# One run of the V products instead of two halves in a fused attention and mixer kernel

## The chip, the cores and the metric

The kernel runs on one core of a Trainium2 chip. The metric is the device time of one execution in microseconds (us), the median over several executions. Short names for the engines: PE is TensorE (PEld its weight loads), DVE is VectorE, ACT is ScalarE, POOL is GpSimd, SP is SyncE. The memories are SBUF and, for what PE writes, the eight banks of PSUM.

## The reference

Attention over 32 heads (batch 4, 8 heads, 576 tokens, head size 64) with a threshold below each row's largest score, then a token mixer and a channel mixer, then a gated convolution layer. The change touches attention alone:

```python
scores = scale * np.matmul(q, k.transpose(0, 1, 3, 2))
thresh = np.max(scores, axis=-1, keepdims=True) - tau
scores = np.where(scores >= thresh, scores, -1000000000.0)
scores = scores - np.max(scores, axis=-1, keepdims=True)
attn = np.exp(scores)
attn = attn / (np.sum(attn, axis=-1, keepdims=True) + 1e-09)
return np.matmul(attn, v).astype(np.float32)
...
x = _moe_ref(x=x, **moe_kwargs)
return _moe2_ref(x=x, **moe2_kwargs)
```

## The kernel before

Every engine has a program of its own, written out by hand, and semaphores tie them together; no planner moves anything. In the first 390 us or so attention and the token mixer are computed, in the rest the channel mixer and the last layer.

Attention goes through 16 pairs of heads. The program calls `body` for k = 0 to 17: body k works on the scores and probabilities of pair k, on the V products of pair k-1 (`at.pv`, k = 1 to 16), and on the token mixer of pair k-2 (`at.mix`, k = 2 to 17). A body has five steps s = 0 to 4, one for each tile of 128 queries; the fifth tile holds the last 64 queries of both heads.

What PE does in step s, in this order: `scores` of the tile two ahead (L979, L981), `turn_probs` of tile s (L998, L1006: the masked probabilities are transposed in pieces into two PSUM banks, `score` 3 and `turn_y`; the second head's pieces wait for that head's mask), `times_v` (L1035, in steps 0 and 1 only), `turn_tails` (L1017), `times_v_tail` (L1045, step 1), token mixer work (steps 2 to 4: L1080, L1089, L1102; L1052 and L1062 turn attention's output), and `score_tails` of the tile three ahead (L967, L970).

`score_tails` writes into the PSUM banks from which DVE reads the scores, so it waits for `max_done`: DVE must have copied the tile before it. DVE does in step s `copy_out` of the tile two ahead (L817: one operation for each head, from PSUM to `negs`, with the row's minimum) and then `mask` of the tile one ahead (L834: one for each head, `negs` and `exps` to `prob`). ACT copies the turned probabilities to SBUF (L596) and takes exponentials (L584). POOL splits arrays into two parts for precise products: `h1h`, `h1l` (L447, L495), `xh`, `xl` (L447, L474), adds `uy` (L502), and splits a piece of a weight, `w1h`, `w1l` (L454, L485); it starts that sequence in step 4, when ACT has written `h1f` (L632). PE's `mix_out` (L1102) in step 4 waits for `h1l`.

`times_v` multiplies the four key tiles of 128 keys (FULL = 4) by V. For each key tile it issues two products of 288 queries (bank `out_t` and bank `mixed`) for each of two heads. Its waits stand ahead of key tile 0 alone.

Of the kernel before, what the change touches and what calls it, by code (L numbers as in the profile page):

```python
# [25 lines left out]
def build(nc, q, k, v, v_tail, tau, w_tok1, w_tok2, w_ch1, w_ch2, w_in, conv_w, w_out, out):  # L26
# [10 lines left out]
    FULL = S // P  # L37
# [155 lines left out]
    with ctx:  # L193
# [763 lines left out]
        def _(pe):  # L957
# [14 lines left out]
            def scores(unit):  # L972

                g, k, t = unit
                par = k % 2
                if t < FULL:
                    for h in range(2):
                        rows = slice(h * D, (h + 1) * D)
                        mm = nc.tensor.matmul(score[:, 2 * h, :], qT[par][rows, t * P:(t + 1) * P], kT[par][rows, 0:MAIN])  # L979
                else:  # L980
                    mm = nc.tensor.matmul(score[:, 0, :], qd[par][:, :], kT[par][:, 0:MAIN])  # L981
                mm.then_inc(s_done, 1)

            def turn_probs(at, t):
                g, k = at.g, at.k
                i = slot_of(k, t)
                if NT * k + t >= 1:
                    pe.wait_ge(turn_drained, 2 * (NT * g + t))
                if t < FULL:
                    for h in range(2):  # L990
                        pe.wait_ge(mask_done, tiles_to(g, t) + h + 1)
                        pe.nop(nofuse=True)
                        for kt in range(FULL):
                            k_at = h * (S + TAIL) + kt * P
                            to = (h * FULL + kt) * D
                            for r in range(2):
                                rows = slice(r * D, (r + 1) * D)
                                mm = nc.tensor.transpose(turn[r][:, to:to + D], prob[rows, i, k_at:k_at + P],  # L998
                                                         ident[rows, rows])
                else:  # L1000
                    pe.wait_ge(mask_done, TILES * (g + 1))
                    pe.nop(nofuse=True)
                    for kt in range(FULL):
                        for r in range(2):
                            rows = slice(r * D, (r + 1) * D)
                            nc.tensor.transpose(turn[r][:, kt * D:(kt + 1) * D], prob[rows, i, kt * P:(kt + 1) * P],  # L1006
                                                ident[rows, rows])
                    to = slice(FULL * D, NT * D)
                    nc.tensor.transpose(turn[0][0:TAIL, to], prob[0:D, i, MAIN:S], ident[0:D, 0:D])
                    mm = nc.tensor.transpose(turn[1][:, to], prob[D:P, i, S - P:S], ident[D:P, D:P])  # L1010
                mm.then_inc(t_done, 1)

            def turn_tails(at, t):
                g, k = at.g, at.k
                if t == 0 and k >= 2:
                    pe.wait_ge(xt_drained, g - 1)
                nc.tensor.transpose(tails[:, t * P:(t + 1) * P], prob[:, slot_of(k, t), MAIN:MAIN + 2 * TAIL], ident[:, :]) \  # L1017
                    .then_inc(tail_turned, 1)

            def times_v(pair, k, kts):  # L1020

                par = k % 2
                if kts[0] == 0:
                    pe.wait_ge(v_loaded[par], V_LOADS * (pair // 2 + 1))
                    pe.wait_ge(turn_drained, 2 * NT * (pair + 1))
                    if k >= 1:
                        pe.wait_ge(x_done, pair)
                        pe.wait_ge(short_x, pair)
                    if k >= 2:
                        pe.wait_ge(u_drained, 2 * (pair - 1))  # L1030
                for kt in kts:
                    for c, bank in enumerate((out_t, mixed)):
                        for h in range(2):
                            mine = slice(h * D, (h + 1) * D)
                            nc.tensor.matmul(bank[mine, 0:HALF], vm[par][:, kt, mine],  # L1035
                                             probT[par][:, h, kt, c * HALF:(c + 1) * HALF],
                                             start=(kt == 0), stop=False, skip_group_check=True)

            def times_v_tail(pair, k):
                par = k % 2  # L1040
                pe.wait_ge(tails_drained, pair + 1)
                if k < 2:
                    pe.wait_ge(set_once, 5)
                for c, bank in enumerate((out_t, mixed)):
                    mm = nc.tensor.matmul(bank[:, 0:HALF], vd[par][:, :], probTt[par][:, c * HALF:(c + 1) * HALF],  # L1045
                                          start=False, stop=True, skip_group_check=True)
                mm.then_inc(pv_done, 1)

            def turn_out(pair):
                pe.wait_ge(out_drained, 2 * (pair + 1))  # L1050
                for t in range(FULL):
                    mm = nc.tensor.transpose(out_t[:, t * P:(t + 1) * P], oT[:, t * P:(t + 1) * P], ident[:, :])  # L1052
                mm.then_inc(xa_done, 1)

            def turn_out_tail(pair):
                nc.tensor.transpose(mixed[:, DT:DT + P], oT[:, MAIN:MAIN + 2 * TAIL], ident[:, :]).then_inc(xa_tail_done, 1)
# [8 lines left out]
            def mix_hidden(pair, k):  # L1065

                if k == 0:
                    pe.wait_ge(wt_split, 3)
                pe.wait_ge(x_split, pair + 1)
                if k < PAIRS - 1:  # L1070
                    pe.wait_ge(out_drained, 2 * (pair + 2))
                else:
                    pe.wait_ge(u_drained, 2 * pair)
                pe.nop(nofuse=True)
                nc.tensor.transpose(mixed[:, DT:DT + TAIL], x32[0:TAIL, FULL, :], ident[0:TAIL, 0:TAIL])
                n = 0
                for kt in range(NT):
                    w = width[kt]
                    for x, wt in ((xh, wt1h), (xh, wt1l), (xl, wt1h)):
                        mm = nc.tensor.matmul(mixed[:, 0:DT], x[0:w, kt, :], wt[0:w, kt, :],  # L1080
                                              start=(n == 0), stop=(n == 3 * NT - 1))
                        n += 1
                mm.then_inc(tok_done, 1)

            def turn_hidden(pair):
                pe.wait_ge(relu_done, pair + 1)
                pe.wait_ge(xt_tail_drained, pair + 1)
                for m in range(KT):
                    mm = nc.tensor.transpose(mixed[:, m * P:(m + 1) * P], h1T[:, m * P:(m + 1) * P], ident[:, :])  # L1089
                mm.then_inc(hT_done, 1)  # L1090
# [53 lines left out]
            def body(at):  # L1144
                g, k = at.g, at.k
                for s in range(NT):
                    two, three = at.unit(s + 2), at.unit(s + 3)
                    if two:
                        scores(two)
                    if at.units:  # L1150
                        turn_probs(at, s)
                    if at.pv and s < 2:
                        times_v(g - 1, k - 1, (2 * s, 2 * s + 1))
                    if at.units and s < FULL:
                        turn_tails(at, s)
                    if at.pv and s == 1:
                        times_v_tail(g - 1, k - 1)
                    if at.mix and s == 2:
                        mix_hidden(g - 2, k - 2)
                        if k == PAIRS + 1:  # L1160
                            hidden(2)
                    if s == 3:
                        if at.mix:
                            turn_hidden(g - 2)
                        if at.pv:
                            turn_out(g - 1)
                            turn_out_tail(g - 1)
                        if k >= PAIRS:
                            hidden(3 * (k - PAIRS))
                    if at.pv and s == 4:  # L1170
                        turn_x(g - 1, k - 1)
                    if at.mix and s == 4:
                        mix_out(g - 2, k - 2)
                        if k == PAIRS:
                            hidden(1)
                    if three:
                        score_tails(three)
# [29 lines left out]
            with pe.Fori(0, B // 2) as j:  # L1207
                for par in range(2):
# [16 lines left out]
                    for kt in range(KF):  # L1225
                        pe.wait_ge(wo_split, kt + 1)
                        pe.wait_ge(z_lo, KF * b + kt + 1)
                        for t in range(FULL):
                            at = slice(t * P, (t + 1) * P)
# [37 lines left out]
```

## Time and profile before

| | |
|---|---|
| median of 3 executions | 900.53 us (900.35 to 900.69) |
| profiled execution | 903.3 us, of which the span of its instructions is 901.5 us |
| PE busy in the span | 849.2 us, 94% |
| DVE, ACT, POOL busy | 430.0, 411.2, 277.9 us |
| mean granted clock of PE | 0.988 of full speed |

The span is the time from the first to the last instruction. A busy time is the time in which at least one instruction of that engine is in flight; PE's matmuls overlap one another, and their ends are modelled.

### The profile page before, as it was taken

The page shows a single profiled execution, that of the slowest core. Times are in us where ns is not written, and L with a number is a line of the kernel's source. Part 1 is how long each engine was busy: PE and PEld are TensorE (multiplying, and loading weights), DVE is VectorE, ACT ScalarE, POOL GpSimd, SP SyncE. Part 2 cuts the span into 40 slices and gives each one's busy share as a digit, 9 for nine tenths or more (in the row PEclk, how much of TensorE's full clock was granted, in tenths as well). Part 3 has the DMA queues.
Part 4 walks back from the last instruction along what each step waited for, and adds up shares of the span by engine and source line. Part 5 has one row for each costly group of instructions (what it writes and reads, how often), then busy time and mean ns, then how long its engine had stood idle before and what let it go on. Part 6 is the DMA issues. An engine that isn't in the chain of part 4 may idle for free.

```text
span 901.5 us, 15052 instructions
## 1 busy us (share of the span) xinstructions
PE 849.2 (94%) x5536; PEld 667.2 (74%) x5536; DVE 430.0 (48%) x839; ACT 411.2 (46%) x866; POOL 277.9 (31%) x218
## 2 busy tenths in 40 slices
PE   4789989999999999979999999999999999999998
PEld 1456666666666666667888888888899989899996
DVE  4877766777777777452121121121121736438290
ACT  2677767777777777532111121121111746447371
POOL 2323332333333333341201010030066463708170
PEclk9799999999999999989999999999999999999999
DMA  7311111111111111300000000000041001010101
GB/s 210 96 44 43 43 45 43 42 42 42 42 42 42 42 42 15 140 1 1 1 0 1 1 1 1 0 1 1 1 152 36 2 1 47 1 58 0 47 0 58
DMA packets 30890, 32.19 MB, mean 36 GB/s; under 512 B 12352, under 2 KB 19072, under 8 KB 30848
## 3 DMA queue, kind: packets, MB, share of 16 engines
q1 hardware_dynamic: 30848, 31.61, 11.8%
q8 instruction: 28, 0.46, 0.2%
q14 instruction: 14, 0.11, 0.0%
HBM read 26.88 MB, written 4.72 MB: 35 GB/s over the span
## 4 chain that ended last, share of the span: by engine, by line
PE 87%; ACT 4%; issue 3%; DVE 2%; POOL 2%; SPq 0%; DMA 0%; ACTq 0%; POOLq 0%; DVEq 0%
PE score L1122 17%; PE score L1218 11%; PE score L979 6%; PE out_t L1137 4%; PE turn_y L1137 4%; PE mixed L1137 4%; PE tails L1137 4%; PE out_t L1035 4%; PE mixed L1080 4%; PE out_t L1203 4%; PE mixed L1035 3%; PE score L998 3%; PE turn_y L1203 2%; PE mixed L1203 2%; PE tails L1203 2%
## 5 line engine op out<-in xcount | busy, mean ns | idle before, releaser
L817 DVE TENSOR_SCALAR_CACHE_REDUCE negs<-score,neg_scale 128x576 f32<-128x576 f32 x144 | 112.7, 816 | 99.7 <-PE score L979 69.7
L895 DVE SCALAR_TENSOR_TENSOR h<-score,h 128x512 fp32r<-128x512 f32 (+1 forms) x60 | 38.3, 638 | 241.7 <-ACT h L676 241.7
L676 ACT ACTIVATE h<-score 128x512 fp32r<-128x512 f32 (+1 forms) x60 | 33.3, 555 | 255.8 <-PE score L1122 255.8
L834 DVE SCALAR_TENSOR_TENSOR prob<-negs,thresh,exps 128x576 f32<-128x576 f32 x144 | 143.1, 1025 | 0.3 <-ACT thresh L587 0.3
L584 ACT ACTIVATE exps<-negs,neg_max 128x576 f32<-128x576 f32 x144 | 104.9, 776 | 6.8 <-DVE negs L817 6.4
L1122 PE MATMUL score<-uh,w1h 128*128 128x512 f32 (+1 forms) x240 | 89.5, 373 | 3.2 <-DVE ul L865 3.2
L1122 PE MATMUL score<-ul,w1h 128*128 128x512 f32 (+1 forms) x240 | 89.1, 371 | 0.0
L1122 PE MATMUL score<-uh,w1l 128*128 128x512 f32 (+1 forms) x240 | 89.0, 371 | 0.0
L552 POOL TENSOR_TENSOR zl<-z,zh 128x512 fp32r<-128x512 f32 x32 | 54.9, 1715 | 98.1 <-ACT zh_t L750 98.1
L979 PE MATMUL score<-kT,qT 64*128 64x512 f32 x256 | 78.9, 695 | 0.0
L998 PEld LDWEIGHTS score<-ident,prob 64*128 64x128 f32 x512 | 43.2, 144 | 45.5 <-issue 45.4
L596 ACT ACTIVATE probT<-score 128x512 f32<-128x512 f32 x64 | 38.2, 598 | 83.6 <-PE turn_y L998 83.6
L447 POOL TENSOR_SCALAR h1h<-h1f 128x256 fp32r<-128x256 f32 x16 | 7.5, 467 | 216.0 <-ACT h1f L632 216.0
L510 POOL TENSOR_TENSOR ul<-uy,uh 128x256 fp32r<-128x256 f32 (+6 forms) x7 | 16.7, 2403 | 173.9 <-ACT uh L663 173.9
L935 DVE SCALAR_TENSOR_TENSOR conv<-hpad,cw,conv 128x576 f32<-128x576 f32 x32 | 27.3, 854 | 77.4 <-ACT conv L763 77.4
L1218 PE MATMUL score<-yl,wih 128*128 128x288 f32 x256 | 54.9, 296 | 0.0
L1218 PE MATMUL score<-yh,wih 128*128 128x288 f32 x256 | 54.8, 296 | 0.0
L1218 PE MATMUL score<-yh,wil 128*128 128x288 f32 x256 | 54.8, 296 | 0.0
L1122 PEld LDWEIGHTS score<-uh,w1h 128*128 128x128 f32 x240 | 45.8, 191 | 11.1 <-issue 3.4
L998 PE MATMUL score<-ident,prob 64*128 64x64 f32 x512 | 47.3, 229 | 4.5 <-DVE prob L834 3.8
L1122 PEld LDWEIGHTS score<-ul,w1h 128*128 128x128 f32 x240 | 45.9, 191 | 7.7
L1122 PEld LDWEIGHTS score<-uh,w1l 128*128 128x128 f32 x240 | 45.7, 191 | 7.7
(184 smaller groups left out, 2050.3 us busy)
## 6 DMA issues: line engine op xcount, KB each, us to landing
qT<-in_q SPq DMA_DIRECT2D x16, 288.0 KB, 2.9
kT<-in_k SPq DMA_DIRECT2D x16, 288.0 KB, 3.0
vm<-in_v SPq DMA_DIRECT2D x16, 256.0 KB, 2.7
result<-ostage SPq DMA_DIRECT2D x16, 256.0 KB, 2.1
w1f<-in_moe_w_ch SPq DMA_DIRECT2D x4, 768.0 KB, 9.2
w2f<-in_moe_w_ch SPq DMA_DIRECT2D x4, 768.0 KB, 7.8
wif<-in_moe_w_in SPq DMA_DIRECT2D x1, 2048.0 KB, 7.8
wof<-in_moe_w_out SPq DMA_DIRECT2D x8, 256.0 KB, 2.5
```

What stands on the lines that cost most here:

```text
L552: nc.gpsimd.tensor_tensor(zl[:, t, :], z32[:, t % 2, 0:MAIN], zh[:, t, :].bitcast(F32), ALU.subtract)
L584: nc.scalar.activation(exps[i][:, h, :], negs[:, i, h, :], ACT.Exp, bias=neg_max[:, i, h:h + 1], scale=-1.0).then_inc(exp_done, 1)
L817: nc.vector.tensor_scalar(negs[:, i, h, :], raw_of[h], neg_scale[:, 0:1], None, ALU.mult, ALU.min, accum_out=neg_max[:, i, h:h + 1]).then_ ...
L834: nc.vector.scalar_tensor_tensor(out=prob[:, i, h * S:(h + 1) * S], in0=negs[:, i, h, :], scalar=thresh[:, i, h:h + 1], in1=exps[i][:, h, ...
L895: nc.vector.scalar_tensor_tensor(out=h3[:, n % RING, 1, 0:w], in0=hidden_banks[n % 4][:, 0:w], scalar=0.0, in1=h3[:, n % RING, 0, 0:w].bit ...
L979: mm = nc.tensor.matmul(score[:, 2 * h, :], qT[par][rows, t * P:(t + 1) * P], kT[par][rows, 0:MAIN])
L998: mm = nc.tensor.transpose(turn[r][:, to:to + D], prob[rows, i, k_at:k_at + P], ident[rows, rows])
L1035: nc.tensor.matmul(bank[mine, 0:HALF], vm[par][:, kt, mine], probT[par][:, h, kt, c * HALF:(c + 1) * HALF], start=(kt == 0), stop=False, s ...
L1122: mm = nc.tensor.matmul(hidden_banks[n % 4][:, 0:w], wt[:, c, kt, :], x[:, kt, 0:w], start=(kt == 0 and i == 0), stop=(kt == KM - 1 and i ...
L1137: mm = nc.tensor.matmul(sum_banks[mt][:, 0:w], wt[:, c, o:o + P], h3[:, n % RING, part, 0:w], start=(c == 0 and i == 0), stop=(c == KC - 1 ...
L1203: mm = nc.tensor.matmul(bank, z, wt[:, kt, :], start=(kt == 0 and n == 0), stop=(kt == KF - 1 and n == 2))
L1218: mm = nc.tensor.matmul(in_banks[c % 2][:, i, 0:HALF], wt[:, kt, c * P:(c + 1) * P], y[:, kt, i * HALF:(i + 1) * HALF], start=(n == 0), st ...
```

## The change

In the body's steps on PE, `times_v` is called once in step 1 with all four key tiles, where it was called in step 0 with the first two and in step 1 with the last two. The products and their number are the same.

```diff
                     if at.units:
                         turn_probs(at, s)
-                    if at.pv and s < 2:
-                        times_v(g - 1, k - 1, (2 * s, 2 * s + 1))
+                    if at.pv and s == 1:
+                        times_v(g - 1, k - 1, range(FULL))
                     if at.units and s < FULL:
                         turn_tails(at, s)
                     if at.pv and s == 1:
```

The instructions of the other four engines keep their order. On PE, steps 0 and 1 of one body (k = 3) stand so before the change; `kd`, `kT`, `qT`, `qd` are the operands of the scores, `ident` with `prob` a transposition of probabilities, `vm` is V, and a row with a wait names the semaphores. Left-out rows are the other pieces of the transpositions and of the V products.

```order
L979 MATMUL score<-kT_69,qT_67 128x512 x2
L998 MATMUL score<-ident,prob 128x64 [waits turn_drained,mask_done]
...
L1035 MATMUL out_t<-probT_77,vm_75 64x288 [waits short_x,x_done,u_drained,turn_drained,v_loaded0]
...
L1017 MATMUL tails<-ident,prob 128x128 [waits xt_drained]
L967 MATMUL score<-kd_84,qT_67 128x2x64 [waits max_done]
L979 MATMUL score<-kT_69,qT_67 128x512 x2
L998 MATMUL score<-ident,prob 128x64 [waits turn_drained,mask_done]
...
L1035 MATMUL out_t<-probT_77,vm_75 64x288 x2
...
L1017 MATMUL tails<-ident,prob 128x128
L1045 MATMUL out_t<-probTt_74,vd_76 128x288 [waits tails_drained]
```

And so after it, the same steps of the same body, with the same rows left out:

```order
L979 MATMUL score<-kT_69,qT_67 128x512 x2
L998 MATMUL score<-ident,prob 128x64 [waits turn_drained,mask_done]
...
L1017 MATMUL tails<-ident,prob 128x128 [waits xt_drained]
L967 MATMUL score<-kd_84,qT_67 128x2x64 [waits max_done]
L979 MATMUL score<-kT_69,qT_67 128x512 x2
L998 MATMUL score<-ident,prob 128x64 [waits turn_drained,mask_done]
...
L1035 MATMUL out_t<-probT_77,vm_75 64x288 [waits short_x,x_done,u_drained,turn_drained,v_loaded0]
...
L1017 MATMUL tails<-ident,prob 128x128
L1045 MATMUL out_t<-probTt_74,vd_76 128x288 [waits tails_drained]
```

The first eight products have moved from between the transpositions of tile 0 and its `tails` to the place behind the transpositions of tile 1, and the five waits of key tile 0 moved with them. The row with `waits max_done` now follows the transpositions of tile 0 with only `tails` in between.

## Rows read from the trace of the kernel before

**Rows 1.** The page: span and busy times, slices of PE's granted clock in tenths.

```profile
span 901.5 us, 15052 instructions
...
PE 849.2 (94%) x5536; PEld 667.2 (74%) x5536; DVE 430.0 (48%) x839; ACT 411.2 (46%) x866; POOL 277.9 (31%) x218
...
PEclk9799999999999999989999999999999999999999
```

**Rows 2.** Busy time by stretch, sum over the five steps of one pair.

```profile
sum 22.55, PE 21.07 PEld 14.10 DVE 16.44 ACT 16.02 POOL 7.66; mean PE 4.21 PEld 2.82 DVE 3.29 ACT 3.20 POOL 1.53
```

**Rows 3.** Waits of that pair, 222.22 to 244.77 us: total, times, longest.

```profile
DVE negs L817 <- PE score L979: 4.1, 3, 2.5
...
PE out_t L1102 <- POOL h1l L495: 1.3, 1, 1.3
```

**Rows 4.** Timeline, PE, steps 0 and 1 of that pair: start, duration, instruction.

```profile
223.78 0.71 PE L1035 MATMUL out_t<-probT,vm 128*64 128x288 f32 x4
...
225.87 0.33 PE L1017 MATMUL tails<-ident,prob 128*128 128x128 f32 x1
226.03 0.39 PE L967 MATMUL score<-kd,qT 128*128 128x128 f32 x2
226.35 1.13 PE L979 MATMUL score<-kT,qT 64*128 64x512 f32 x4
227.31 0.22 PE L998 MATMUL score<-ident,prob 64*128 64x64 f32 x1
...
227.77 0.24 PE L998 MATMUL score<-ident,prob 64*128 64x64 f32 x1
...
228.16 0.71 PE L1035 MATMUL out_t<-probT,vm 128*64 128x288 f32 x4
...
229.67 0.66 PE L1035 MATMUL mixed<-probT,vm 128*64 128x288 f32 x4
230.25 0.33 PE L1017 MATMUL tails<-ident,prob 128*128 128x128 f32 x1
```

**Rows 5.** Timeline, DVE, the same steps.

```profile
223.40 0.82 DVE L817 TENSOR_SCALAR_CACHE_REDUCE negs<-score,neg_scale 128x576 f32<-128x576 f32 x1 [1.43 <-PE score L979]
...
224.88 0.08 DVE L817 DVE_READ_ACCUMULATOR negs<-score,neg_scale 128x1 f32 x1
224.88 1.26 DVE L834 SCALAR_TENSOR_TENSOR prob<-negs,thresh,exps 128x576 f32<-128x576 f32 x1
...
226.07 1.54 DVE L834 SCALAR_TENSOR_TENSOR prob<-negs,thresh,exps 128x576 f32<-128x576 f32 x1
227.54 0.08 DVE L834 DVE_READ_ACCUMULATOR prob<-negs,thresh,exps 128x1 f32 x1
227.77 0.82 DVE L817 TENSOR_SCALAR_CACHE_REDUCE negs<-score,neg_scale 128x576 f32<-128x576 f32 x1
```

**Rows 6.** Timeline, POOL, from step 4 of the pair before on.

```profile
218.79 0.41 POOL L447 TENSOR_SCALAR h1h<-h1f 128x256 fp32r<-128x256 f32 x1 [14.43 <-ACT h1f L632]
...
224.69 0.83 POOL L454 TENSOR_TENSOR w1h<-w1f,ones 128x384 f32 x1
225.68 1.32 POOL L485 TENSOR_TENSOR w1l<-w1f,w1h  x1 [0.15 <-POOL w1h L454]
```

**Rows 7.** Timeline, DVE: second mask of tile 1, first and last like it.

```profile
88.29 1.54 DVE L834 SCALAR_TENSOR_TENSOR prob<-negs,thresh,exps 128x576 f32<-128x576 f32 x1
...
361.69 1.54 DVE L834 SCALAR_TENSOR_TENSOR prob<-negs,thresh,exps 128x576 f32<-128x576 f32 x1
```

**Rows 8.** Timeline, body k = 1: PE, then DVE.

```profile
46.37 0.39 PE L967 MATMUL score<-kd,qT 128*128 128x128 f32 x2
...
48.23 0.71 PE L1035 MATMUL out_t<-probT,vm 128*64 128x288 f32 x4
...
44.51 0.81 DVE L817 TENSOR_SCALAR_CACHE_REDUCE negs<-score,neg_scale 128x576 f32<-128x576 f32 x1
...
45.98 0.81 DVE L834 SCALAR_TENSOR_TENSOR prob<-negs,thresh,exps 128x576 f32<-128x576 f32 x1
```

**Rows 9.** Timeline, DVE: second mask of tile 1, last of the short ones.

```profile
135.35 0.82 DVE L834 SCALAR_TENSOR_TENSOR prob<-negs,thresh,exps 128x576 f32<-128x576 f32 x1
```

**Rows 10.** PE's longest wait before 390 us, and the stretch behind it.

```profile
128.45 0.40 PE L1102 MATMUL out_t<-wt2h,h1h 128*128 128x288 f32 x1 [2.16 <-POOL h1l L495]
...
129.65:133.06 3.41, 3.41 (x15) 2.05 (x16) 0.00 (x0) 0.93 (x3) 3.26 (x3) 0.51 0.00 0
```

## The prediction

> **What bounds the kernel now.** I read the page first, for the bound: PE is busy for 849 of 901.5 us, at full clock nearly throughout [rows 1]. Then the busy time by stretch, for a pair of the steady part of attention: PE works 21.1 of 22.55 us, DVE 16.4, ACT 16.0 [rows 2]. Then the waits of the same pair, for what PE's missing 1.5 us are: 1.3 us of it is one wait in step 4, for POOL's `h1l` [rows 3]. DVE waits 4.1 us for scores in the same pair, so over a whole pair PE is the slower one [rows 3]. That says what an instruction taken out of PE would bring; it doesn't say what one moved within PE costs. For that one has to set the timelines of PE, DVE and POOL side by side in the two steps [rows 4 to 6].
>
> The reader is to see there a chain that runs beside PE's. Scores of tile 2 end, and DVE copies them out from 223.40 to 224.96 (224.88 and the 0.08 of the accumulator's read). Then come the two masks of tile 1, ready at 227.62 [rows 5]. PE needs the first result for `score_tails`, which starts at 226.03, so it is 1.07 us early. It needs the last one for the second half of the transpositions of tile 1, which starts at 227.77, 0.15 us behind the mask: here PE is waiting already [rows 4, 5]. So between the start of the V products of step 0 (223.78) and 227.77, DVE is the bound, and the first half of the V products lies in time that PE would otherwise wait.
>
> DVE's chain is long there because of its masks: 1.26 and 1.54 us [rows 5] where a mask elsewhere takes 0.81 [rows 8]. Each of the two ends soon after a POOL operation that was running when it started (`w1h`, 224.69 to 225.52, and `w1l`, 225.68 to 227.00) [rows 6]. The 1.54 stands in 12 of the 15 bodies that have both masks and V products (k = 3, 4 and 6 to 15; 88.29 is the first and 361.69 the last) [rows 7]. In k = 1, 2 and 5 the second mask takes 0.81 or 0.82 [rows 8, 9].
>
> **The change, part by part.** Nothing is added or removed: 32 products of each body stay. Body 16 has V products but no scores or transpositions of its own, so there the two calls stood one behind the other and nothing moves: 15 bodies are changed.
>
> *Step 0 gets shorter, but not by what is taken out.* From the first product to `tails` the first half takes 225.87 - 223.78 = 2.09 us [rows 4]. Without it `tails` could go at 223.78 and `score_tails` 0.16 us later, at 223.94. But it waits for the copy of tile 2, ready at 224.96. It goes about 0.1 us behind that, at 225.05, and step 1 begins 226.03 - 225.05, about 1.0 us, sooner than before, with about 1 us of new idle time.
>
> *Step 1, the 12 bodies with long masks.* The transpositions of tile 1 would start at 227.31 - 1.0 = 226.3. Their first half takes about 0.4 us and then they wait for the mask, ready at 227.62: the second half starts at 227.77 as before, and the whole gain of step 0 is lost, in a second gap of about 1 us. The mask itself doesn't come sooner. Its chain starts when the scores of tile 2 are there, of which nothing has changed, and goes on through DVE without a gap. The POOL operations that hold it start from ACT's `h1f` in the step before [rows 6]. Behind the transpositions the V products start at 228.16 as before, and now there are twice as many. A half takes 2.09 us with its start; a group of four goes on every 0.485 us (from 228.16 to 229.67 are three of them and 0.05 of start) [rows 4], so the second half adds 4 x 0.485 = 1.94 us. I take 1.94. The bounds are 1.9 and 2.09, the latter if a start is paid twice. All that follows on PE (`tails`, the tail of V, the scores of the last tile) is 1.94 us later.
>
> *Does anything behind it take the delay up?* The waits that follow are DVE's for scores, ACT's for transpositions, POOL's for `h1f`, and PE's for `h1l` [rows 3, 6]. `h1f` is ACT's copy of a PE result of step 3, so `h1l` moves with PE, and the wait in step 4 stays 1.3 us. DVE is ahead and only waits longer. V's load for the next pair waits for `pv_done`, 2 us later, in a period of 22.55. I find nothing that takes it up. `turn_tails` of step 0 also waits for ACT's copy out of `tails`; that copy is of the step before and doesn't become the last.
>
> 12 x 1.94 = 23.3 us (22.8 to 25.1).
>
> *The three bodies with short masks.* In k = 1 the copy of tile 2 is done at 44.51 + 0.81 = 45.32 and `score_tails` started at 46.37 [rows 8], so step 0 gains 1.0 us as above. The second mask is done at 45.98 + 0.81 = 46.79. Half a set of transpositions stands 0.4 us before 48.23 - 0.4, that is, the second half started near 47.85, and may now start near 46.9: the 1.0 us is kept. So the body costs 1.94 - 1.0 = 0.94 us; k = 2 and 5 likewise. Together 2.8 us (0 to 6.3, the ends being a gain kept in full and one lost in full).
>
> *The clock.* The changed bodies have two idle stretches of about 1 us within 4 us. Before 390 us one wait of 2.16 us on PE stands in the trace, and behind it the granted clock is 0.51 for 3.41 us [rows 10], the lower of the two levels (1.2 for 2.4 GHz). The waits of 1.3 us in the other bodies left it at full. Two gaps of together 2 us, with 1.7 us of work in between, lie between these rows, and nearer to the 2.16. Such a stretch costs half its work: at most 1.7 us. None at all gives 0, one in each of the 12 bodies gives 20. Since the gaps are split I take one or two drops in the 12 bodies, 2 us.
>
> Sum: 23.3 + 2.8 + 2 = 28.1 us. The profiled execution was 903.3 us, with a span of 901.5; it would become about 931.4. On the median of 900.5, which is 2.8 us below it, I expect **928.5 us**, 3.1% slower.
>
> **The rivals.**
>
> *Drops of the clock in many bodies.* The place is the run of V products in step 1, right behind the two gaps. For it speaks the one drop that the trace shows; against it, that each of the two gaps alone is shorter than the 1.3 us which left the clock at full. If 8 of the 12 drop, at 1.5 us: 26.1 + 12 = 38 us, 938.5 us; all of them reach 946. The Trainium skill ("TensorE: Matmul & The Clock Gate", "A second HAM failure mode: psum-queue depth-cycling") tells of a kernel in which frequent short idles between groups of matmuls keep sending the clock to its lower level. By that rule this rival would be the likely one; the 1.3 us wait that every body has already, at full clock, does not bear the rule out so far. Chance 0.14.
>
> *The masks are no longer held.* If POOL's operations and the masks fell apart, each mask would take 0.81, the chain would be 0.45 + 0.73 = 1.2 us shorter, and all bodies would cost what k = 1 does: 15 x 0.94 = 14 us, 914.5 us. Against it: neither POOL's start nor the masks' depends on anything that moved. Chance 0.08.
>
> *The delay is taken up in step 4.* If PE's 1.3 us wait for `h1l` shrank by the delay, a long body would cost 1.94 - 1.3 = 0.64 us and a short one nothing: 8 us, 908.5 us. It would take an `h1l` that does not depend on PE's step 3. Taken up altogether it is no change. Chance 0.05 for the first, 0.03 for the second.
>
> *Faster: the order of PE's work is free.* If PE never waited for the copy and the mask, the run would save one start in each body, 2.09 - 1.94 = 0.15 us: 15 x 0.15 = 2.3 us, 898.3 us. It decides if DVE's chain from 223.40 to 227.62 were more than 2.09 us shorter than it is; the masks would have to give up 1.2 us to POOL and 0.9 us besides. Chance 0.03.
>
> **How the numbers follow.** The forecast (23 to 31 us, 923.5 to 932) has 0.67, the rivals 0.14, 0.08, 0.05, 0.03 and 0.03. The range reaches from 921 to 936: it holds the forecast's own range, the case of doubled starts, and up to six drops of the clock. What is left out is about a third of the clock's rival (0.05), the 914.5, the 908.5 and the two below, 0.24 together; that is near enough to 2 in 10, and reaching for 914.5 would widen the range by a third for 0.08. A change under 0.2% (1.8 us) can't be told from none in this kernel; slower by more has 0.94, within it 0.03, faster 0.03.
>
> **What the profile after would show.** In step 0, `tails` right behind the transpositions and a wait of about 1 us at L967 for DVE's `negs`. In step 1, the transpositions waiting about 1 us for `prob` at L834, with masks still at 1.26 and 1.54 us. V products as one run of 4.0 us. Wait at L1102 for `h1l` still 1.2 to 1.4 us. A pair takes 24.5 us in place of 22.55. DVE waits some 2 us longer for the scores of the last tile. Everything behind attention is as before, only later. I would be wrong if the masks changed their length, if the wait at L1102 shrank, or if the granted clock showed a lower level in body after body.

## The result: 3% slower, and the profile after

The changed kernel takes 928.2 us (median of 4 executions, 927.8 to 928.7) where the kernel before takes 900.6 (4 executions, 900.4 to 901.3): a ratio of 1.0305, with an interval of 1.0288 to 1.0323. The forecast was 928.5 us, in a range of 921 to 936.

The page of the profiled execution (928.7 us), first the span and the busy times, then the slices of PE and of its granted clock:

```profile
span 926.9 us, 15057 instructions
...
PE 850.5 (92%) x5536; PEld 669.3 (72%) x5536; DVE 429.4 (46%) x839; ACT 411.2 (44%) x866; POOL 277.7 (30%) x218
...
PE   4788888888888888879999999999999999999998
...
PEclk9999999999999999998999999999999999999999
```

Against [rows 1] the work is the same: PE is busy 1.3 us more of 850 and with weight loads 2.1 us more of 667, the other engines no more than before. PE has become less busy where attention runs. The granted clock has a 9 in the second slice, the highest digit, where it was a 7 before.

The waits of one steady body (k = 9, the one of [rows 3]; 233.28 to 257.86 us): total, times, longest.

```profile
DVE negs L817 <- PE score L981: 3.9, 1, 3.9
...
PE out_t L1102 <- POOL h1l L495: 1.3, 1, 1.3
PE score L967 <- DVE negs L817: 1.1, 2, 0.9
PE score L998 <- DVE prob L834: 1.0, 1, 1.0
```

Two waits of PE are new against [rows 3], 0.9 us for the copy and 1.0 for the mask; the one for `h1l` has stayed at 1.3. The timeline of PE in steps 0 and 1 of that body, from the scores of tile 2 on:

```profile
233.28 1.13 PE L979 MATMUL score<-kT,qT 64*128 64x512 f32 x4
...
234.83 0.33 PE L1017 MATMUL tails<-ident,prob 128*128 128x128 f32 x1
236.07 0.49 PE L967 MATMUL score<-kd,qT 128*128 128x128 f32 x2 [0.92 <-DVE negs L817]
236.49 1.13 PE L979 MATMUL score<-kT,qT 64*128 64x512 f32 x4
...
238.82 0.25 PE L998 MATMUL score<-ident,prob 64*128 64x64 f32 x1 [0.96 <-DVE prob L834]
...
239.31 0.71 PE L1035 MATMUL out_t<-probT,vm 128*64 128x288 f32 x4
...
243.34 0.33 PE L1017 MATMUL tails<-ident,prob 128*128 128x128 f32 x1
```

And DVE there:

```profile
234.46 0.82 DVE L817 TENSOR_SCALAR_CACHE_REDUCE negs<-score,neg_scale 128x576 f32<-128x576 f32 x1 [1.42 <-PE score L979]
...
235.94 1.26 DVE L834 SCALAR_TENSOR_TENSOR prob<-negs,thresh,exps 128x576 f32<-128x576 f32 x1
...
237.12 1.54 DVE L834 SCALAR_TENSOR_TENSOR prob<-negs,thresh,exps 128x576 f32<-128x576 f32 x1
238.60 0.08 DVE L834 DVE_READ_ACCUMULATOR prob<-negs,thresh,exps 128x1 f32 x1
```

DVE's part is [rows 5] again, with the same durations: 4.22 us from its first copy (234.46) to the second mask (238.68), as from 223.40 to 227.62 before. PE's second half of the transpositions starts 238.82 - 233.28 = 5.54 us behind the scores of tile 2; before it was 227.77 - 222.22 = 5.55. The 2.09 us of V products that PE had in between are gone from there, and the second half of the transpositions came no sooner for it. The run of products then takes 243.34 - 239.31 = 4.03 us where a half took 2.09.

### The profile page after: what moved, and what is told of

Its sections match the earlier page's. It is cut to its first block, busy times and chain, and to the rows that moved or that the text cites. A ratio compares the mean times of both kernels' runs of the same rounds, so it can differ in the third digit from the quotient of the medians.

```text
span 926.9 us, 15057 instructions
## 1 busy us (share of the span) xinstructions
PE 850.5 (92%) x5536; PEld 669.3 (72%) x5536; DVE 429.4 (46%) x839; ACT 411.2 (44%) x866; POOL 277.7 (30%) x218
## 4 chain that ended last, share of the span: by engine, by line
PE 81%; DVE 7%; ACT 4%; issue 4%; POOL 2%; DMA 0%; SPq 0%; ACTq 0%; DVEq 0%; POOLq 0%
PE score L1122 16%; PE score L1218 11%; PE score L979 4%; DVE prob L834 4%; PE out_t L1137 4%; PE turn_y L1137 4%; PE mixed L1137 4%; PE tails L1137 4%; PE mixed L1080 4%; PE out_t L1035 4%; PE out_t L1203 4%; PE mixed L1035 3%; DVE negs L817 2%; PE turn_y L1203 2%; PE mixed L1203 2%
## 5 line engine op out<-in xcount | busy, mean ns | idle before, releaser
L979 PE MATMUL score<-kT,qT 64*128 64x512 f32 x256 | 77.0, 680 | 0.0
L967 PE MATMUL score<-kd,qT 128*128 128x128 f32 x128 | 31.0, 325 | 33.1 <-DVE negs L817 24.1
L967 PEld LDWEIGHTS score<-kd,qT 128*128 128x128 f32 x128 | 20.3, 197 | 45.2 <-DVE negs L817 34.0
```

The lines of the kernel that those rows point to most:

```text
L967: nc.tensor.matmul(raw_tails, qT[par][:, t * P:(t + 1) * P], kd[par][:, :].rearrange("p (n c) -> p n c", c=TAIL))
```

## The experiments

Each ran beside the kernel before on the same chip. The period is the time from the tail-of-V products (L1045) of one body to those of the next, read from the timeline of PE, here the mean over the bodies between 205 and 343 us before and the like stretch of the others: 22.61 us before, 24.62 in the changed kernel. The two kernels with half of V leave out key tiles 2 and 3; they are there for their time alone.

| kernel | median, us | ratio to before | interval | period, us |
|---|---|---|---|---|
| half of V, in step 1 only | 896.9 | 0.9972 | 0.9953 to 0.9991 | 22.68 |
| all of V in step 0 | 899.8 | 0.9991 | 0.9975 to 1.0008 | 22.51 |
| changed, w1 split moved | 912.8 | 1.0145 | 1.0114 to 1.0175 | 23.39 |
| before, w1 split moved | 895.5 | 0.9947 | 0.9929 to 0.9966 | 22.27 |
| half of V, in step 0 only | 873.0 | 0.9695 | 0.9678 to 0.9712 | 20.82 |
| one key tile in step 0, three in step 1 | 912.4 | 1.0144 | 1.0115 to 1.0174 | 23.57 |
| three in step 0, one in step 1 | 897.1 | 0.9968 | 0.9955 to 0.9980 | 22.31 |
| w1 split moved, all of V in step 0 | 898.1 | 0.9975 | 0.9964 to 0.9986 | 22.45 |

The kernel before had medians of 900.9 us beside the first four and 899.9 beside the last four.

**Half of the products, in step 1 only.**

```diff
-                    if at.pv and s < 2:
-                        times_v(g - 1, k - 1, (2 * s, 2 * s + 1))
+                    if at.pv and s == 1:
+                        times_v(g - 1, k - 1, (0, 1))
```

> This kernel leaves out the products of key tiles 2 and 3 in every body and multiplies tiles 0 and 1 in step 1, nothing in step 0: 16 of 32 V products of each body are gone. Theory A (the first half of the V products lay in time that PE would otherwise wait for DVE's copy and masks): taking it away saves nothing in the 12 bodies with long masks and about 1.0 us in each of the others, so about 897.5 to 900.5 us. Rival B (PE's work is the bound, each product counts): 15 x 2.09 = 31 us less, about 869 us.

Measured: 896.9 us, a little under the range of theory A. (The trace shows each V product as two matmuls, so the 16 of 32 in the text above are 8 of the 16 products that the program issues in a body.) Of the 2.09 us taken out of each body, nothing is saved in the steady ones; their period is even 0.07 us longer. The waits of one body (219.6 to 242.3 us):

```profile
PE out_t L1102 <- POOL h1l L495: 1.3, 1, 1.3
PE score L967 <- DVE negs L817: 1.1, 2, 0.9
PE score L998 <- DVE prob L834: 0.9, 1, 0.9
```

They are the waits of the changed kernel: PE idles where it multiplied. Rival B is out. What is saved lies in body 1 (0.89 us), body 2 (0.96 us) and body 16 (1.95 us), together 3.8 us, of which the longer steady periods take some 0.8 back.

**Half of the products, in step 0 only.** The same with `s == 0`.

> This kernel leaves out the same products as the one with half of V in step 1 only (key tiles 2 and 3), but keeps tiles 0 and 1 in step 0 and has nothing in step 1. Theory A (the half in step 0 is cover, the half in step 1 is on the path): the removed 1.94 us count in full where nothing else waits, so up to 15 x 1.94 = 29 us less, about 872 us; DVE's copy of tile 3 and the masks of tile 2 may give up to 0.5 us of it back in each body, 880 us. Rival B (it does not matter which half goes): the same time as that kernel, 897 us.

Measured: 873.0 us, 27 us less than before, with a period 1.79 us shorter. The same number of products left out in the one place gives 27 us and in the other 4. The waits of one body (212.5 to 233.3 us):

```profile
PE out_t L1102 <- POOL h1l L495: 1.3, 1, 1.3
...
PEld score L970 <- DVE negs L817: 0.4, 1, 0.4
...
PE score L967 <- DVE negs L817: 0.2, 1, 0.2
```

A small wait of the weight load for DVE's copy of tile 3 (L970) appears. The scores of the last tile (L981) start 0.85 us behind the last products of the tail of V (234.26 to 235.11), where it was 0.65 before (230.91 to 231.56). These 0.20 us are of the size by which 1.79 falls short of 1.94.

**One key tile in step 0, three in step 1.** `times_v(g - 1, k - 1, ((0,), (1, 2, 3))[s])`.

> Key tile 0 in step 0, tiles 1 to 3 in step 1. Theory A (what is moved out of step 0 is exposed in full in the 13 bodies with long masks, and not at all in bodies 1 and 2 while DVE's copy is no later than PE): 13 x 1.0 = 13 us, 913.6 us, a period of 23.6 us, a gap ahead of the masks only and none ahead of the copy. Rival F (the second gap alone costs, or only both gaps together): 900.6 us or 928 us.

Measured: 912.4 us, a period of 23.57. PE in this kernel, step 1 of a body:

```profile
230.88 0.25 PE L998 MATMUL score<-ident,prob 64*128 64x64 f32 x1 [0.97 <-DVE prob L834]
...
231.28 0.71 PE L1035 MATMUL out_t<-probT,vm 128*64 128x288 f32 x4
```

The wait ahead of the copy is not there, as expected, and the one ahead of the mask is 0.97 us, as large as with all four tiles in step 1. The loss is 0.96 us in a body, half of the change's 2.01. So it counts how much stands in step 0, and one gap alone has a price: rival F, with 900.6 or 928 us, is out.

**Three in step 0, one in step 1.** `times_v(g - 1, k - 1, ((0, 1, 2), (3,))[s])`.

> Key tiles 0 to 2 in step 0, tile 3 in step 1. Theory A (cover beyond DVE's chain brings nothing but the 0.1 to 0.2 us of the mask wait that is there now): 898 to 900 us. Rival G (each tile that stands earlier is worth about 1 us in each body, on this side too): 887 us.

Measured: 897.1 us, 0.32% faster than before, a period 0.30 us shorter, about 1 us under the range of theory A and far from G's 887. A tile more or less in step 0 is worth 0.96 us on one side of the kernel before and 0.30 on the other. The 0.30 is more than the 0.1 to 0.2 expected because the wait for the mask cost PE more than the 0.15 us by which the transpositions follow the mask: from the scores of tile 3 to the V products of step 1 PE took 1.81 us before (226.35 to 228.16 in [rows 4]; 1.85 in the next body) and takes 1.55 in this kernel (224.44 to 225.99), where it doesn't wait.

**All four in step 0.** `if at.pv and s == 0: times_v(g - 1, k - 1, range(FULL))`.

> All four key tiles in step 0, none in step 1. Theory A (it matters what covers DVE's chain of step 0, and step 1 has cover of its own): no loss; one start of 0.15 us and the 0.2 us for which PE waited for the mask before are saved, about 896 to 899 us. Rival C (a long run in one step costs as such, wherever it stands, because DVE gets its scores late): slower by about 28 us, as the change is, 928 us.

Measured: 899.8 us, no difference from before that the interval tells (0.9975 to 1.0008), a period 0.10 us shorter. A run of four is not what costs: rival C is out. Theory A's 896 to 899 was too low. Up to the tail of V a body is 0.42 us shorter, the start and the mask wait saved: from the first V product to L1045 PE takes 6.22 us (222.54 to 228.76), and before it took 6.64 (223.78 to 230.42). But behind it some 0.3 us are lost again. In step 1 PE now has little between the scores of tile 3 and those of the last tile, and its weight load waits for DVE's copy of tile 3 there, 0.4 us a body; the scores of the last tile start 0.87 us behind the last products of the tail of V, where it was 0.65. The rest is lost in steps 2 and 3.

**POOL's split of w1 moved, in the changed kernel.** It ran beside the masks of tile 1; now it starts behind the scores of the last tile.

```diff
                 g = at.g
+                if at.units:
+                    pool.wait_ge(s_done, NT * (g + 1))
+                    split_w1(g)
                 if at.mix:
                     split_hidden(g - 2)
...
-                if at.units:
-                    split_w1(g)
```

> The changed kernel, with POOL's split of a piece of w1 moved to the front of its body and made to wait for the scores of the last tile (step 2 on PE), where before it ran beside the masks of tile 1. Theory A with the masks held by POOL: masks of tile 1 at 0.8 us each, the second gap of a body nearly gone, each of 13 bodies about 1.05 us shorter: 928.2 - 13.7 = 914.5 us. Rival D (the masks are long for another reason, or the second gap comes from something else): 928 us.

Measured: 912.8 us, a period 1.23 us shorter than that of the changed kernel. DVE in this kernel, where 228.92 and 229.66 are the masks of tile 1, and 238.28 and 239.15 those of tile 3, beside which the split now runs (lines are one higher here):

```profile
228.92 0.81 DVE L835 SCALAR_TENSOR_TENSOR prob<-negs,thresh,exps 128x576 f32<-128x576 f32 x1
229.66 0.81 DVE L835 SCALAR_TENSOR_TENSOR prob<-negs,thresh,exps 128x576 f32<-128x576 f32 x1
...
238.28 0.94 DVE L835 SCALAR_TENSOR_TENSOR prob<-negs,thresh,exps 128x576 f32<-128x576 f32 x1
239.15 1.57 DVE L835 SCALAR_TENSOR_TENSOR prob<-negs,thresh,exps 128x576 f32<-128x576 f32 x1
```

The masks of tile 1 fall to 0.81 us, and the masks beside which POOL now works take on the length. POOL's two operations hold whatever mask starts beside them. Each held mask ends 0.61 or 0.62 us behind the end of the POOL operation that ran when it started (`w1h` ends at 238.61 and `w1l` at 240.10 here, the masks at 239.22 and 240.72; in [rows 5, 6] 225.52 and 227.00, and 226.14 and 227.61). PE's wait for the mask is gone and the one for the copy stays:

```profile
229.06 0.49 PE L968 MATMUL score<-kd,qT 128*128 128x128 f32 x2 [0.92 <-DVE negs L818]
```

Rival D is out. The 1.23 us are not all of the change's cost, for the same move makes the kernel before shorter too, by 0.34 us a body (next experiment). With short masks the change costs 23.39 - 22.27 = 1.12 us in a steady body, with held ones 2.01. So 0.9 of the 2.0 us hang on the held masks; the other 1.1 us are there without them, with the wait for the copy.

**The same in the kernel before.**

> The same move of POOL's split in the kernel before. Theory A: the chain of DVE is 1.2 us shorter but was covered all but 0.2 us, so 12 x 0.2 = 2.4 us at most is gained: 898 to 900.5 us, if the masks of step 2 and 3, now beside the split, have slack. Rival D: no change, 900.6 us, with masks as long as before.

Measured: 895.5 us, 2.5 us under the range, 0.53% faster than before (interval 0.34 to 0.71%) and the lowest median of the kernels that compute everything. Its period is 0.34 us shorter, more than the 0.2 expected: here too PE takes 1.55 us from the scores of tile 3 to the V products (220.97 to 222.52), 0.26 less than before. Besides, the period between bodies 4 and 5 is 22.27 us, where the kernel before had 24.75 in its profiled execution (see the end). The masks of tile 1 in this kernel:

```profile
223.63 0.81 DVE L835 SCALAR_TENSOR_TENSOR prob<-negs,thresh,exps 128x576 f32<-128x576 f32 x1
...
224.37 0.82 DVE L835 SCALAR_TENSOR_TENSOR prob<-negs,thresh,exps 128x576 f32<-128x576 f32 x1
```

**Both, the moved split and all of V in step 0.**

> POOL's split of w1 moved as in the kernel that ran faster than the kernel before, and all four key tiles in step 0. Theory A: both small gains add up where they are not the same wait: 0.34 us of a body from the split, 0.1 to 0.15 from the single start: 893.5 to 895.5 us. Rival H (both remove the same wait): 895.5 us or a little above.

Measured: 898.1 us, 0.25% faster than before; both expectations were too low, H by less. With the moved split alone it was 0.53%; the two intervals just touch, and the period tells them apart, 22.45 us against 22.27, near the 22.51 of all-in-step-0 without the move. In both kernels with V in step 0 a weight load waits 0.4 us for DVE's copy of tile 3. By the timelines one start of 0.15 us is saved against the moved split alone, 0.21 us are lost between the tail of V and the scores of the last tile (0.86 us in place of 0.65) and 0.12 us in steps 2 and 3, which makes the 0.18. That the wait for the copy is the cause of the 0.21 was not tried by itself.

## Why the prediction was right

*Step 0 shorter by 1.0 us, with a gap of 1 us ahead of the copy.* Shown: 0.92 us of wait; the scores of tile 3 start 236.49 - 233.28 = 3.21 us behind those of tile 2, where it was 226.35 - 222.22 = 4.13 [rows 4], so 0.92 us were gained. The prediction had 1.0, since it took the scores of tile 3 to follow `score_tails` after 0.32 us as before (226.03 to 226.35); behind the wait it is 0.42 (236.07 to 236.49).

*A second gap of about 1 us for the mask, which loses it again.* Shown: 0.96 us, at a mask that ends as before. Moving POOL's split takes this gap away, and with it 1.2 us of the body, so the hold of the masks, argued from [rows 5, 6], is shown by experiment. One reading beside it was wrong: that a mask elsewhere takes 0.81 us. In the kernel before, the two masks of step 4 are held as well, beside `h1l` and `xh`, at 1.15 and 1.26 us in the pair of [rows 3]:

```profile
219.62 1.15 DVE L834 SCALAR_TENSOR_TENSOR prob<-negs,thresh,exps 128x576 f32<-128x576 f32 x1
```

*The second half added in full, 1.94 us.* The run takes 4.03 us, as worked out. A steady body became 24.62 - 22.61 = 2.01 us longer, 0.07 more than the sum: the products start 0.49 us behind the second half of the transpositions (238.82 to 239.31) where it was 0.39.

*Nothing behind it takes the delay up.* The wait for `h1l` is 1.3 us as before, and DVE's for the scores of the last tile 3.9 us, 2.0 more.

*The short-mask bodies at 0.94 us.* Body 1 cost 1.1 us by its distance to the start (42.49 to 50.49 us before, 39.64 to 48.70 after). With POOL's split moved all bodies have short masks, and there the change costs 912.8 - 895.5 = 17.3 us, 1.15 for each of 15 bodies; so 0.94 was 0.2 too low. Body 5 did not stay short: its second mask now takes 1.55 us. Before, the clock had dropped ahead of it [rows 9, 10], and the scores came late against POOL's split. The other traces bear that out but for one: with a drop there the mask takes 0.81 or 0.82 us (half in step 0, three then one), without it 1.54 or 1.55 (half in step 1, one then three); all four in step 0 has a drop and 1.55. So 13 bodies cost 2.0 and two about 1: 28 us against 26.1 in the forecast's two terms.

*The clock, 2 us.* This term was mis-sized, and its reason wrong. In the profiled execution not one of the 13 bodies with two gaps has a stretch at the lower level. There is one in body 2, behind a wait of 1.12 us for a mask and one of 0.79 for the copy, with 0.7 us of work in between:

```profile
63.65:67.06 3.41, 3.41 (x24) 1.87 (x26) 2.30 (x7) 1.61 (x5) 0.00 (x0) 0.52 0.00 0
```

The trace of the kernel before had such a pair of waits too, and the prediction, which speaks of one wait of 2.16 us, left it out:

```profile
28.09 0.25 PE L998 MATMUL score<-ident,prob 64*128 64x64 f32 x1 [1.15 <-DVE prob L834]
...
29.60 0.43 PE L970 MATMUL score<-kT,qd 128*128 128x64 f32 x2 [0.78 <-DVE negs L817]
...
30.72:40.96 10.24, 9.16 (x57) 5.31 (x56) 6.53 (x16) 5.54 (x13) 0.62 (x1) 0.50 0.22 66
```

This is the 7 in the second slice of [rows 1]. In the profiled execution after, the two waits are 0.69 and 0.41 us, the clock stays at full, and body 1 begins 2.85 us sooner. The stretch of [rows 10] is at full clock too, though the wait that stood ahead of it has stayed (2.16 also is not the longest wait on PE: the first matmul waits 8.89 us):

```profile
133.04 0.40 PE L1102 MATMUL out_t<-wt2h,h1h 128*128 128x288 f32 x1 [2.16 <-POOL h1l L495]
```

So the premise that a wait of 2.16 us brings the clock down and one of 1.3 us doesn't was drawn from one case, and the changed kernel contradicts it. In the profiled pair the spans differ by 25.4 us: about 28 of the bodies and 1.5 for the drop in body 2, less 2.85 at the start and 1.5 for the drop that body 5 no longer has, and 0.5 us behind attention. The medians differ by 27.6. The mean granted clock of the four executions of the changed kernel was 0.993 to 0.996, no lower than in the executions of the kernel before (0.988 to 0.998 in 25 of them): the rival in which many bodies drop did not happen in any. Which of the possible places drops differs from one execution to the next, and nothing here says what decides it. The terms that were too small (1.9 us) and the clock's 2 us, which did not come, cancel: part of the closeness of 928.5 to 928.2 is luck.

## What to carry to other kernels

An engine that is 94% busy can still depend on a chain of another engine at one place, and work that stands there is free as far as that chain is the longer. Set the two timelines side by side from the instruction that starts the chain to the one that waits for its end. Work moved out of that stretch cost its full length here (0.96 us for one key tile, 2.01 for two), and work taken out of it brought nothing. To see which it is, leave the work out in the one place and in the other: here the same products were worth 4 us and 27.

## What the runs showed of the hardware that was not expected

- A mask on DVE (two SBUF inputs, 128x576) takes 0.81 us alone and 0.9 to 1.6 us (2.10 in body 2, beside `xl` of 2.06) where a POOL operation is running when it starts, and the length follows POOL's operations when they move to other masks. In the traces of before, changed, three-then-one and both kernels with the split moved and V not all in step 0, each such mask ends 0.59 to 0.63 us behind that operation, and the others take 0.76 to 0.82 us; a mask that starts with under 0.15 us of the operation left takes 0.8 us too. A POOL operation that starts while a mask runs did not hold it (`w1l` at 225.68, the mask from 224.88 to 226.14). `copy_out`, which reads PSUM, takes 0.82 and 0.81 us also where POOL's `uy` runs beside it (from 223.40 and 224.15; `uy` from 223.32 to 224.74). The Trainium skill ("GPSIMD Engine Reference", "8. Key points") says that GpSimd shares its SBUF interfaces with VectorE, with contention for Vector instructions that have two SBUF inputs; the rows agree that such masks are held. How long they are held comes from the rows alone.
- Between bodies 4 and 5 one period is 24.75 us before, with an `h1l` of 1.25 us on POOL in place of 0.72, the 2.16 us wait and the stretch at the lower clock of [rows 10]. In the changed kernel, where the clock stays up there, the same wait makes the period 25.21 us in place of 24.62. So the longer `h1l` costs some 0.6 us and the clock's drop the other 1.5. In the three kernels with the moved split `h1l` takes 0.72 there and the period is like the others (22.27, 23.38 and 22.44 us). Body 4 is the first of the program's loop; why the one operation is longer there was not tried.
- The same waits did not always bring the clock down. Body 4's wait of 2.16 us has a stretch at the lower level at its end or within 1.3 us behind it in the profiles of four kernels (before, all in step 0, half in step 0, three then one) and none in three (changed, half in step 1, one then three). The pair of 1.12 to 1.14 and 0.78 to 0.79 us in body 2, with 0.7 us of work in between, was followed by one in two (changed; changed with the split moved) and by none in one (half in step 1). In the changed kernel two waits of 0.9 to 1.0 us (in one body 0.9 and 0.6) with 1.8 us of work in between left the clock at its upper level in all 13 bodies that have them.
